# One small product block moved in front of an MLP half on TensorE

## The reference, cut to what matters

```python
for t in range(S):                       # S = 768 tokens, B = 4, H = 8 heads, D = 48
    cur = einsum('bhd,bhe->bhde', u * k[t], v[t])
    y[t] = einsum('bhd,bhde->bhe', r[t], state + cur)
    state = w[t] * state + einsum('bhd,bhe->bhde', k[t], v[t])
x = y as (3072 tokens, 384)
g = elu(x @ w_in);        x = g @ w_out      # d_ff = 2048
g = h * sigmoid(1.702 h), h = x @ w2_in;     return g @ w2_out
```

## Time and profile before

| | |
|---|---|
| median of 3 executions | 976.77 us (976.70 to 979.65) |
| the profiled execution | 978.74 us |
| its span, first to last instruction | 976.9 us |
| TensorE busy | 937.8 us (96%) |
| VectorE, ScalarE, GpSimd busy | 546.7, 456.1, 67.6 us |
| mean granted clock of TensorE | 0.986 |

### The profile page before, as it was taken

How to read it: one execution, slowest core, us unless ns; L and a number is a source line. 1 busy time by engine, 2 the same in 40 slices (tenths; PEclk the granted TensorE clock), 3 DMA queues, 4 the chain that set the end, 5 groups by cost and what they waited for, 6 DMA issues and landing times.

```text
span 976.9 us, 27105 instructions
## 1 busy us (share of the span) xinstructions
PE 937.8 (96%) x11872; PEld 912.9 (93%) x11872; DVE 546.7 (56%) x915; ACT 456.1 (47%) x874; POOL 67.6 (7%) x81
## 2 busy tenths in 40 slices
PE   4589999999999999999999999999999999999998
PEld 4479999999899899999999999999999999999998
DVE  8878686685675766866844444343433344333333
ACT  2547637546456355374455764333333333333332
POOL 1261000000000000000000641000000000000000
PEclk8799999999999999999999999999999999999999
DMA  6443211211402212113005510000000000000000
GB/s 186 106 137 91 57 52 26 65 44 28 105 3 56 76 26 56 52 25 82 3 7 201 201 53 1 25 1 24 0 25 0 24 0 20 4 1 25 1 25 25
DMA packets 15798, 47.30 MB, mean 48 GB/s; under 512 B 2864, under 2 KB 6832, under 8 KB 15696
## 3 DMA queue, kind: packets, MB, share of 16 engines
q1 hardware_dynamic: 13680, 40.85, 14.9%
q0 software_dynamic: 1536, 4.50, 1.6%
q10 hardware_dynamic: 480, 0.40, 0.2%
HBM read 35.71 MB, written 8.85 MB: 46 GB/s over the span
## 4 chain that ended last, share of the span: by engine, by line
PE 95%; issue 2%; DVE 2%; DMA 1%; ACT 0%; ACTq 0%; DVEq 0%
PE psum L1288 42%; PE psum L1301 42%; PE psum L1058 4%; PE psum L1020 1%; PE psum L1172 1%; PE psum L1136 1%; PE psum L1164 1%; PE psum L1101 1%; PE psum L1094 1%; DVE arena L708 0%; DVE blocks L762 0%; DMA x_raw<-y 0%; DMA arena<-k_channels_dram 0%; DVE arena L702 0%; PE psum L1067 0%
## 5 line engine op out<-in xcount | busy, mean ns | idle before, releaser
L1288 PE MATMUL psum<-x_hi,w_split 128*128 128x384 f32 x1536 | 395.6, 338 | 2.7 <-issue 2.7
L1301 PE MATMUL psum<-g_hi,w_split 128*128 128x384 f32 x1536 | 392.0, 336 | 0.0
L1288 PEld LDWEIGHTS psum<-x_hi,w_split 128*128 128x128 f32 x1536 | 281.4, 189 | 3.6 <-issue 3.6
L1301 PEld LDWEIGHTS psum<-g_hi,w_split 128*128 128x128 f32 x1536 | 277.6, 188 | 0.0
L1288 PE MATMUL psum<-x_lo,w_split 128*128 128x384 f32 x768 | 263.9, 344 | 5.9 <-DVE x_lo L799 4.4
L1301 PE MATMUL psum<-g_lo,w_split 128*128 128x384 f32 x768 | 261.6, 341 | 0.2 <-issue 0.2
L507 ACT ACTIVATE g_hi<-gate 128x384 fp32r<-128x384 f32 x256 | 134.5, 525 | 170.6 <-DVE gate L818 88.1
L823 DVE TENSOR_TENSOR g_lo<-gate,g_hi 128x384 fp32r<-128x384 f32 x256 | 143.6, 561 | 118.3 <-ACT g_hi L507 118.3
L816 DVE TENSOR_TENSOR gate<-expo,psum 128x384 f32<-128x384 f32 x128 | 70.8, 553 | 162.6 <-ACT expo L503 162.6
L1288 PEld LDWEIGHTS psum<-x_lo,w_split 128*128 128x128 f32 x768 | 144.6, 188 | 7.9 <-issue 7.0
L1301 PEld LDWEIGHTS psum<-g_lo,w_split 128*128 128x128 f32 x768 | 144.5, 188 | 3.0 <-issue 0.7
(11 more groups left out here) (94 smaller groups left out, 449.2 us busy)
## 6 DMA issues: line engine op xcount, KB each, us to landing
v_sb<-v_tokens_dram SPq DMA_DIRECT2D x8, 576.0 KB, 5.7
arena<-w_channels_dram SPq DMA_DIRECT2D x14, 288.0 KB, 5.0
arena<-k_channels_dram SPq DMA_DIRECT2D x14, 288.0 KB, 4.4
arena<-r_channels_dram SPq DMA_DIRECT2D x14, 288.0 KB, 4.6
x_scratch<-x_sb SPq DMA_DIRECT2D x7, 576.0 KB, 3.3
arena<-x_scratch SPq DMA_DIRECT2D x1, 4032.0 KB, 12.8
staging<-weights_dram SPq DMA_DIRECT2D x9, 384.0 KB, 3.6
blocks<-weights_dram SPq DMA_DIRECT2D x9, 384.0 KB, 3.7
```

Source lines behind the costliest of these rows:

```text
L1288: mm = pe.matmul(hidden(f), w_tile(f, lo, m * P), xx, start=n == 0, stop=n == 3 * KT - 1)
L1301: mm = pe.matmul(acc(to, m), w_tile(f, lo, (KT + m) * P), gg, start=f == 0 and n == 0, stop=f == NF - 1 and n == 2)
```

## The change

One line moves: `near(1)` stands in front of `up(0, 0, 0)`, and parts 0 and 1 of the first MLP tile follow one another. Nothing is added or removed, and the orders of the other engines are the same.

```diff
                 keys_values(0, 0)
                 first_outputs()
+                near(1)
                 up(0, 0, 0)
-                near(1)
                 up(0, 0, 1)
                 step(0, 1, 1, 0, 0)
```

## The result

The changed kernel takes 981.03 us (median of 11 executions; one of them, at 1041.57 us, was disturbed and is left out of the comparison, the others lie between 979.40 and 983.07), the kernel before 977.90 us beside it (11 executions). The ratio is 1.0035, with a 95% interval of 1.0023 to 1.0046: 3.4 us slower, 2.2 to 4.5 (the difference of the two medians is 3.1).

A forecast was written before the change was run, and what follows sets the result against it. TensorE is 95% of the kernel, but around the move VectorE's fixed order, waiting on part 0, sets the pace. +1.4, +4.1, -1.6 and -1.55 give +2.4 us, 979.2 on the median; range 976.6 to 980.9.

The forecast's parts named there:

- TensorE idle longer for r: Before step 1's first MLP half, TensorE resumes at 49.3 when r lands, against 47.89 before: +1.4 us.
- near in front of part 0: On TensorE, near runs from 49.3 to 53.4 at the granted clock, ahead of part 0: +4.1 us.
- VectorE's idle time gone: VectorE's idle time between its gated(0, 0) work and gated(0, 1), spent waiting for part 1, disappears: -1.55 us.
- Step 1: Near cannot use TensorE's idle 4.43 us: r lands at 49.3, x_lo released TensorE at 47.89; 1.4 us more idle.
- Steps 2 to 4: TensorE: near 4.3 us at half clock or 2.5 full, part 0 3.22 or 1.58; part 0 likeliest ends at 55.0.
- early bound: TensorE's full clock comes 2.5 us after it resumes, at 51.8; part 0 ends at 54.4, delay +1.8 us, 978.6.
- likeliest case: TensorE's full clock comes 3.9 us after it resumes, from 53.2; near ends at 53.4, part 0 at 55.0.
- The rival of a clock that stays at half through part 0: TensorE not granted full clock until part 0 is nearly through: delay 4.1 us, time 980.9; chance 0.26.
- Step 5: VectorE's fixed order: gated(0, 0) 1.17 us after part 0, gated(0, 1) 4.74 later at 60.9; part 1's stall hidden.
- Step 6: From gated(0, 1) on, everything shifts whole by 2.4 us; idle before level 2 grows from 0.78 to 1.8, level 3's stays.
- Early r: r is there at 45.4, so near fills TensorE's idle time; gated(0, 1) 1.9 us earlier, time 974.9; chance 0.05.
- No delay at all: Something later than the moved lines has slack that takes up the 2.4 us; time 976.8; chance 0.13.

The follow-up runs named there:

- e15: The kernel before, unchanged, run again for a third profile, in an execution whose step 0 ended late; ratio 0.9995.
- e13: Kernel before, with SyncE issuing r and v of step 1 only after the six small transfers into x_raw have landed; ratio 0.9999 against before.
- e4: Changed kernel, with VectorE's pick_diag(1, 0) and grow_r(1, 1) before gated(0, 0), and grow_k(1, 1) before gate_lo(0, 0); ratio 1.0009 against before.
- e3: Changed kernel, with near(1) reading split weights instead of r, so not waiting for r (another computation); ratio 0.9975 against before, 2.4 us faster.
- e8: Changed kernel with the edits of e3 and e4 together; ratio 0.9975 against before, 2.4 us below.
- e5: Kernel before, with 12 extra unread products on TensorE behind step 0's last output product; ratio 1.0072 against before, 7 us slower.
- e6: Changed kernel, with 16 extra unread products on TensorE behind step 0's last output product; ratio 1.0122 against before, 12 us slower.

## Why the prediction was wrong

Over all comparisons the changed kernel has a median of 980.45 us (42 executions) and before 977.82 (149): 2.6 us slower. The cause, the direction and the place were as forecast; two sizes were not, the base and the wait for r. The delay as a whole, 2.4 us, came out near what was measured (2.6 over all, 3.1 to 3.4 in the first comparison), but in part by luck: against an execution of before whose step 0 ends late its first term is 1.1 us too small, and the term for near is 0.2 to 0.6 too large over the four profiles of the changed kernel. The changed kernel's profile laid against the two kinds of before:

| term of the sum | forecast | against before | against e15 |
|---|---|---|---|
| TensorE idle longer for r | +1.4 | +1.31 | +2.49 |
| near in front of part 0 | +4.1 | +3.48 | +3.48 |
| part 0 at the full clock | -1.6 | -1.39 | -1.39 |
| VectorE's idle time gone | -1.55 | -1.66 | -1.30 |
| `gated(0, 1)` later by | 2.4 | 1.75 | 3.28 |

- **The base.** "The median of the three is 2.0 us lower than this execution, so on the median 979.2": three executions gave 976.77, the eleven beside the changed kernel 977.90, and all 149 give 977.82. So 1.1 us of the 1.8 between 979.2 and 981.03 are the base, and the range, built from cases of the mechanism, had no room for it. On the base of 977.90 the same 2.4 us would have given 980.3, inside the range. Of the 2.0 us that the profiled execution lay above the three, some 1.4 may be the half clock at 509 us, far from this place; the executions without a profile don't show whether they had it.
- **Step 1, the wait for r: the mechanism right, the size of its difference off.** Near starts 5.53 to 5.87 us behind step 0 and is released by r, as worked out (5.84). But "+1.4, TensorE idle longer for r" took part 0's start of before from one profile, 4.43 us, in which the small transfers had themselves been slowed by r. Where they are not, it is 3.25, and the term is +2.5 (5.74 - 3.25). In all four of its profiles the changed order pays r's landing (an idle time of 5.53 to 5.87 us); the order of before pays 1.2 to 1.35 us of slowed small transfers in two of three and nothing in the third. e13 and e15 show both halves of this.
- **Steps 2 to 4, near and the clock: right.** Near took 3.6 to 4.0 us from its start to its end (forecast 4.1), and part 0 1.8 (1.6). In the changed kernel's profile the full clock came between 54.5 and 54.7, some 2.6 to 2.8 us after TensorE came back at 51.95, between the early bound (2.5) and the likeliest case (3.9) and nearer to the bound. The rival of a clock that stays at half through part 0 was seen in none of the four profiles, and their executions, 979.5 to 980.7 us, are slow without it; so it isn't needed for the time.
- **Step 5, VectorE: right.** From part 0's end to `gated(0, 0)` 1.18 us (1.17), from there to `gated(0, 1)` 4.64 (4.74), with the idle time of 1.55 us gone. The stall in part 1 is gone too: four products into it TensorE goes on without an idle time. e4 shows that this order is what hands the delay on.
- **Step 6: right in its result, wrong in a detail.** Level 2 and level 3 are shifted alike (23.97 and 30.66 against 22.24 and 28.94), and the rest gets no longer. But the idle time in front of level 2 is 0.44 us and not 1.8: a stall of 0.84 us falls into the products between the levels (one packet of instructions is moved from 64.9 to 66.2 us, the stall ends at 67.67), and these take 5.1 us without it and not 4.8. It isn't on the path, since level 2 waits for `grow_k(1, 2)` in any case.
- **The rivals.** Early r (stood in for by e3, where near doesn't read r at all): 2.4 us faster, where 1.9 had been worked out. No delay at all: excluded by the times, and no stretch behind level 3 makes anything up.

What stays open: why e3 with VectorE's better order (e8) gains nothing more, why TensorE waits longer behind level 3 in e5 and e6, and the clock's own share in the scatter between executions (974.54 to 981.12 us for before). No order tried beat the kernel before, except those that read other data in place of r.

## What to carry to other kernels

Idle time in front of an instruction is room only for work whose last input is there; look for its landing time, not for the size of the gap, and then ask what is queued behind. And before a term is taken as a difference of two moments of one profile, ask what else released the earlier one: here it hung on the same transfer, and in one of three profiles it was 1.2 us earlier. A median of three is no base for a forecast of 0.3%.

## What the runs showed of the hardware that I had not expected

TensorE's instruction stream has borders at fixed counts: five kernels with different work in front stall behind the same 205th product (1.68, 2.79, 2.84, 2.94 and, with part 1 in the middle of near, 0.26 us), and one and the same kernel stalls there for 0.28 to 1.68 us in three executions. Twelve extra products in an idle time made the kernel 7 us slower. And where two loads of 288 KB and one of 576 KB were issued 1.3 to 1.5 us behind the first of six transfers of 24 KB, the slowest of the six took 3.7 to 4.1 us, against 2.3 where they were issued 2.3 us behind it and 2.8 where they waited for all six.
